# Attention with sinks and two feed-forward layers in one kernel: first tiles' splits, tiny sums, the sinks' values and the last store rearranged

## What is computed

```python
keep = is_sink | in_window            # 4 sinks, window of 128
scores = np.where(keep, scores, -1000000000.0)
a = np.exp(scores - max); a = a / (np.sum(a, axis=-1, keepdims=True) + 1e-09)
x = a @ v                             # batch 2, 8 heads, 768 positions, 64 per head
h = x @ w_in                          # 1536 tokens, 512 -> 1024
sm = e / (np.sum(e, axis=-1, keepdims=True) + 1e-09)      # e = exp(h - h_max)
solu = h * sm
ln = (solu - mu) / np.sqrt(var + 1e-06) * g_ln
x2 = ln @ w_out                       # 1024 -> 512
r = np.maximum(x2 @ w2_in, 0.0)       # 512 -> 2048
out = (r * r) @ w2_out                # 2048 -> 512
```

## Time and profile before

| what | value |
|---|---|
| runs shown | 488.4, 488.94 (median), 490.08 us |
| profiled execution's own time | 489.99 us |
| its span in the trace | 488.0 us |
| PE busy | 474.4 us (97%) |
| DVE busy | 289.5 us (59%) |
| ACT busy | 202.9 us (42%) |
| POOL busy | 95.4 us (20%) |
| DMA moved | 40.75 MB |

### The profile page before, as it was taken

How to read it: one execution, slowest core, us unless ns; L and a number is a source line. 1 busy time by engine, 2 the same in 40 slices (tenths; PEclk the granted TensorE clock), 3 DMA queues, 4 the chain that set the end, 5 groups by cost and what they waited for, 6 DMA issues and landing times.

```text
span 488.0 us, 7178 instructions
## 1 busy us (share of the span) xinstructions
PE 474.4 (97%) x2580; PEld 386.6 (79%) x2580; DVE 289.5 (59%) x528; ACT 202.9 (42%) x531; POOL 95.4 (20%) x138
## 2 busy tenths in 40 slices
PE   7989988999999999999999999999999999999997
PEld 5657767887888888888888888888888888888885
DVE  3999999999999999576655453422223232322232
ACT  3767557655776566323225342422222222222221
POOL 2456043020302330719940000000000000000000
PEclk9999999999999999999999999999999999999999
DMA  8921426675558334196400000200000010000002
GB/s 239 311 54 55 145 59 199 172 211 174 153 162 206 95 103 130 27 263 218 97 1 0 0 1 0 88 0 0 0 0 0 0 63 23 1 0 0 1 1 87
DMA packets 50150, 40.75 MB, mean 84 GB/s; under 512 B 27912, under 2 KB 36104, under 8 KB 49608
## 3 DMA queue, kind: packets, MB, share of 16 engines
q1 hardware_dynamic: 49656, 39.83, 28.0%
q10 hardware_dynamic: 464, 0.53, 0.4%
HBM read 29.86 MB, written 10.49 MB: 83 GB/s over the span
## 4 chain that ended last, share of the span: by engine, by line
PE 85%; DVE 9%; issue 2%; ACT 1%; POOL 1%; DMA 1%; SPq 0%; DVEq 0%; POOLq 0%; ACTq 0%
PE score_ps L1524 27%; PE h_ps L1538 13%; PE w_ps L1365 12%; PE h_ps L1325 10%; PE wt_ps L1538 7%; PE w_ps L1538 7%; PE o_ps L1295 3%; PE score_ps L1267 2%; PE wt_ps L1275 2%; DMA x2T<-kT 1%; PE o_ps L1312 1%; PE wt_ps L1267 1%; DVE nmax L931 1%; DVE prob L996 1%; DVE sm L919 1%
## 5 line engine op out<-in xcount | busy, mean ns | idle before, releaser
L1524 PE MATMUL score_ps<-x2T_hi,w2in_hi 128*128 (+1 forms) x192 | 74.8, 389 | 0.0
L1524 PE MATMUL score_ps<-x2T_hi,w2in_lo 128*128 (+1 forms) x192 | 74.7, 389 | 0.0
L1524 PE MATMUL score_ps<-x2T_lo,w2in_hi 128*128 (+1 forms) x192 | 74.7, 389 | 0.0
L1198 DVE TENSOR_TENSOR e<-e 128x512 f32<-128x512 f32 x24 | 17.1, 712 | 82.1 <-ACT e L865 82.1
L1198 DVE TENSOR_TENSOR sq<-relu 128x512 f32<-128x512 f32 x24 | 17.7, 738 | 77.9 <-ACT relu L865 77.9
L865 ACT ACTIVATE relu<-score_ps 128x512 f32<-128x512 f32 x24 | 14.4, 598 | 94.2 <-PE score_ps L1524 94.2
L865 ACT ACTIVATE e<-score_ps 128x512 f32<-128x512 f32 x24 | 14.4, 599 | 92.5 <-PE score_ps L1524 92.5
L1524 PEld LDWEIGHTS score_ps<-x2T_hi,w2in_lo 128*128 128x128 f32 x192 | 36.1, 188 | 7.5
L1524 PEld LDWEIGHTS score_ps<-x2T_hi,w2in_hi 128*128 128x128 f32 x192 | 36.0, 188 | 7.5
L1524 PEld LDWEIGHTS score_ps<-x2T_lo,w2in_hi 128*128 128x128 f32 x192 | 36.0, 188 | 7.5
L675 ACT ACTIVATE prob<-sm,nbias 128x132 f32<-128x132 f32 (+1 forms) x96 | 37.7, 394 | 0.8
(11 more groups left out here) (185 smaller groups left out, 1096.6 us busy)
## 6 DMA issues: line engine op xcount, KB each, us to landing
w2in<-w_in SPq DMA_DIRECT2D x4, 1024.0 KB, 5.2
u_dram<-uT SPq DMA_DIRECT2D x16, 256.0 KB, 3.3
lnT_raw<-u_dram SPq DMA_DIRECT2D x32, 128.0 KB, 2.6
w2out<-w_out SPq DMA_DIRECT2D x8, 512.0 KB, 8.0
V<-v SPq DMA_DIRECT2D x12, 256.0 KB, 3.3
x2T<-x_dram SPq DMA_DIRECT2D x12, 256.0 KB, 4.6
x_dram<-x SPq DMA_DIRECT2D x44, 64.0 KB, 2.3
k_raw<-kT SPq DMA_DIRECT2D x20, 132.0 KB, 2.8
```

The costliest lines, as they stand in the source:

```text
L1198: nc.vector.tensor_tensor(sq[f % 2], relu[f % 2], relu[f % 2], ALU.mult).then_inc(sq_ready, 1)
L1524: done = mm(h2_ps[f % 2], ws[:, c, fs], xs[:, c, bass.ts(blk, BLK)], start=(c == 0 and i == 0), stop=(c == MC - 1 and i == 2))
```

## The change

What it does, by engine:

- **SP** loads the fourth part of w_in ahead of the sinks' values.
- **ACT** rounds this part before the last copy of tile 1's scores. It takes over the rounding of tile 2's queries and keys from POOL. For every tile it computes hz and hz_eps in two activations on 128x1 (`hidden_sum`), behind the exponentials of h.
- **DVE** splits tile 1's keys only after tile 0's maxima of h, and tile 2's keys between the two gates of tile 0. Its three tiny operations per tile are gone.
- **POOL** computes var in front of rstd (`inverse_std`).
- **PE** takes the sinks' values ahead of the first scores of a step and of the other values, for tiles 3 to 5 and 7 to 11. They now open the accumulation in o_ps, and the rounding of x waits for both kinds. ACT's and POOL's first work of stage B waits for the other values where it waited for the sinks'.
- **The end:** the last block's stores are written out behind the loop; the last tile is copied in halves, of which SP stores one and ACT the other.

```diff
...
+def sinks_lead(n):
...
+    return has_sinks(n) and n > EARLY
...
         minus_half = sbt("minus_half", [P, 1])
+        z_floor = sbt("z_floor", [P, 1])
...
         y_done, y_copied_act, y_copied_dve = sem("y_done"), sem("y_copied_act"), sem("y_copied_dve")
+        y_end_copied = sem("y_end_copied")
...
             load_w_in(2)
+            load_w_in(3)
             load_v_sink(0)
-            load_w_in(3)
...
             load_x2T(2)
-            with sp.Fori(0, NB) as blk:
+            with sp.Fori(0, NB - 1) as blk:
...
                     sp.dma_start(out[bass.ds(blk * BLK + i * P, P), :], y[i]).then_inc(y_stored, 16)
-            sp.wait_ge(y_stored, 16 * TB * NB)
+            for i in range(TB):
+                cols = slice(0, DM // 2 if i == TB - 1 else DM)
+                sp.wait_ge((y_copied_act, y_copied_dve)[i % 2], TB // 2 * (NB - 1) + i // 2 + 1)
+                sp.dma_start(out[(NB - 1) * BLK + i * P:(NB - 1) * BLK + (i + 1) * P, cols], y[i][:, cols]
+                             ).then_inc(y_stored, 16)
+            sp.wait_ge(y_stored, 16 * (TB * NB + 1))
...
             nc.gpsimd.memset(minus_half[:, :], -0.5).then_inc(built, 1)
+            nc.gpsimd.memset(z_floor[:, :], SM_EPS * LN_EPS ** 0.5).then_inc(built, 1)
...
             def inverse_std(t):
+                pool.wait_ge(moments_ready, t + 1)
+                pool.wait_ge(hz_eps_ready, t + 1)
+                nc.gpsimd.tensor_tensor(var[:, :], moments[:, 1:2], hz_eps[:, :], ALU.add).then_inc(var_ready, 1)
...
-            def round_k(n):
-                pool.wait_ge(k_loaded, 32 * (n - 1))
-                pool.wait_ge(k_split, n - 1)
-                nc.gpsimd.tensor_copy(KH[:, :, KEYS_SINKS[n % 2]], raw_keys(n)).then_inc(k_hi, 1)
...
             round_v_sink(0)
-            round_k(2)
-            round_q(2)
...
             halves(1, 1)
+            pool.wait_ge(q_hi, 1)
...
-            pool.wait_ge(o_done, sink_tiles(NT))
+            pool.wait_ge(pv_done, GROUPS * NT)
...
+            def hidden_sum(t):
...
+                act.wait_ge(h_exped, 2 * t + 2)
+                nc.scalar.activation(hz[:, :], hsum[:, 0:1], ACT.Identity, bias=hsum[:, 1:2], scale=1.0
+                                     ).then_inc(hz_ready, 1)
+                act.wait_ge(hz_ready, t + 1)
+                if t:
+                    act.wait_ge(var_ready, t)
+                else:
+                    act.wait_ge(built, 3)
+                nc.scalar.activation(hz_eps[:, :], hz[:, :], ACT.Square, bias=z_floor[:, :], scale=LN_EPS ** 0.5
+                                     ).then_inc(hz_eps_ready, 1)
...
                     act.wait_ge(o_done, sink_tiles(n) + 1)
-                else:
-                    act.wait_ge(pv_done, GROUPS * n + GROUPS)
+                act.wait_ge(pv_done, GROUPS * n + GROUPS)
...
                     hidden_exp(t + 1)
+                    hidden_sum(t + 1)
...
                     hidden_exp(t + 1)
+                    hidden_sum(t + 1)
...
                 copy_sinksT(2)
+                hidden_sum(1)
...
             copy_earlier(1, 2)
+            round_w_in(3)
...
                 softmax_exp(1, h)
-            round_w_in(3)
...
             copy_pT(1, 0)
+            round_q(2)
...
             copy_sinksT(1)
+            round_k(2)
+            hidden_sum(0)
...
             act.wait_ge(lnT_split, len(LN_PARTS) * (NT - 2))
-            act.wait_ge(o_done, sink_tiles(NT))
+            act.wait_ge(pv_done, GROUPS * NT)
...
             hidden_exp(NT - 1)
+            hidden_sum(NT - 1)
...
                 copy_y(blk)
+            act.wait_ge(y_end_copied, 1)
+            act.dma_start(out[T - P:T, DM // 2:DM], y[TB - 1][:, DM // 2:DM]).then_inc(y_stored, 16)
...
                 nc.vector.tensor_tensor(u[:, cols], h_ps[:, cols], e[:, cols], ALU.mult).then_inc(u_ready, 1)
-                if half == 1:
-                    nc.vector.scalar_tensor_tensor(hz[:, :], hsum[:, 0:1], SM_EPS, hsum[:, 1:2], ALU.add,
-                                                   ALU.add).then_inc(hz_ready, 1)
...
-            def variance(t):
-                dve.wait_ge(hz_ready, t + 1)
+            def aggregate(t):
                 dve.wait_ge(bstat_ready, 2 * t + 2)
-                nc.vector.scalar_tensor_tensor(hz_eps[:, :], hz[:, :], LN_EPS, hz[:, :], ALU.mult, ALU.mult
-                                               ).then_inc(hz_eps_ready, 1)
                 nc.vector.bn_aggr(moments[:, :], bstat[:, :, :]).then_inc(moments_ready, 1)
-                dve.wait_ge(hz_eps_ready, t + 1)
-                dve.wait_ge(moments_ready, t + 1)
-                nc.vector.tensor_tensor(var[:, :], moments[:, 1:2], hz_eps[:, :], ALU.add).then_inc(var_ready, 1)
...
                     stats(t, half)
-                variance(t)
+                aggregate(t)
...
                 gate(0, 0)
+                split_k(2)
...
                 stats(0, 1)
-                variance(0)
+                aggregate(0)
...
                 stats(1, 1)
-                variance(1)
+                aggregate(1)
...
             row_max(1, 1)
-            split_k(1)
...
             hidden_max_all(0)
-            split_k(2)
+            split_k(1)
...
                     dve.wait_ge(y_done, TB * blk + i + 1)
-                    nc.vector.tensor_copy(y[i], y_ps[i]).then_inc(y_copied_dve, 1)
+                    if blk == NB - 1 and i == TB - 1:
+                        nc.vector.tensor_copy(y[i][:, 0:DM // 2], y_ps[i][:, 0:DM // 2]).then_inc(y_copied_dve, 1)
+                        nc.vector.tensor_copy(y[i][:, DM // 2:DM], y_ps[i][:, DM // 2:DM]).then_inc(y_end_copied, 1)
+                    else:
+                        nc.vector.tensor_copy(y[i], y_ps[i]).then_inc(y_copied_dve, 1)
...
                         last = mm(o_ps[rows, cols], V[:, slot, h * D:(h + 1) * D], pT[:, g, j * P:(j + 1) * P],
-                                  start=(g == 0 and part == 0 and i < 2),
-                                  stop=(alone(n) and g == GROUPS - 1 and i >= HG - 2), skip_group_check=True)
+                                  start=(g == 0 and part == 0 and i < 2 and not sinks_lead(n)),
+                                  stop=((alone(n) or sinks_lead(n)) and g == GROUPS - 1 and part == len(parts) - 1 and i >= HG - 2), skip_group_check=True)
...
                 pe.wait_ge(p_sinkT_copied, sink_tiles(n) + 1)
+                if sinks_lead(n):
+                    pe.wait_ge(xT_split, n)
...
                     cols = slice(c * P, (c + 1) * P)
-                    last = mm(o_ps[:, cols], v_sink[0:SKS, n // TPB, cols], p_sinkT[0:SKS, :], start=False,
-                              stop=(c == MC - 1), skip_group_check=True)
+                    last = mm(o_ps[:, cols], v_sink[0:SKS, n // TPB, cols], p_sinkT[0:SKS, :],
+                              start=(c == 0 and sinks_lead(n)), stop=(c == MC - 1 and not sinks_lead(n)), skip_group_check=True)
...
                 first = LEAD if t == EARLY else 0
+                if has_sinks(n):
+                    sink_values(n)
...
                 values(n, 1)
-                if has_sinks(n):
-                    sink_values(n)
...
                 n = NT - 1
+                sink_values(n)
...
                 values(n, 1)
-                sink_values(n)
...
```

## The result

The changed kernel took 487.09 us (median of 7 runs, 486.21 to 488.67) where the kernel before took 489.54 in the same comparison (488.4 to 490.23). The ratio is 0.9946, with a 95% interval of 0.993 to 0.9963, which leaves out 1: faster, by 0.54%. The prediction was 486.7 us, between 485.3 and 488.4. The profiled execution took 487.09 us, with a span of 485.4.

What follows compares the result with a forecast made beforehand. PE was taken to bound stage B and the steady steps, DVE the first tiles. Gains of 1.0 + 0.35 + 0.4 + 0.35 + 0.1 = 2.2 us took the median from 488.94 to 486.7 us, range 485.3 to 488.4.

Steps and rivals of the forecast that it cites:

- steady steps: Tiles 4, 5, 7 to 10: fewer stops between forms of product save 0.4 us, bounds 0 and 1.0.
- Part 1: First tiles: the new order of loads, roundings and splits brings tile 1's hidden product 1.0 us earlier, bounds 0.3 and 1.8.
- step 2: Sinks' values fill PE's wait for tile 4's keys, with DVE's tiny sums gone: 0.35 us, bounds 0 and 0.59.
- Rival (a): First tiles give nothing, as DVE's wait for ACT's key rounding or POOL's longer chain takes it; 487.7 us, chance 0.20.
- Part 2, steady steps: Moving tiny sums to ACT and POOL only gives DVE slack in steady steps, since PE is the bound: nothing gained.
- u at 69.98 not 0.5 but 0.35 earlier, held by POOL: In step 2, DVE's merge comes about 0.5 us earlier, but u only 0.35, held by POOL.
- Parts 2 and 3 are both needed there: In step 2, the moved tiny sums and the sinks' values ahead give 0.35 us only together.
- I take 0.06 a step: Steady steps: of PEld's 0.17 us idle ahead of the sinks, part is hidden; 0.06 us saved in each of six steps.
- Rival (c): More gain: PEld's whole 0.17 us goes in six steady steps, first tiles give 1.7; 485.4 us, chance 0.12.
- Rival (b): Slower: DVE's chain, with 0.09 us of slack left, becomes the bound of the steady steps; 490.6 us, chance 0.08.
- Last step: Sinks fill PEld's 0.39 us wait for POOL's mask before tile 11's last values: 0.35 us, bounds 0.15 and 0.5.
- Tail: Last tile in halves, its stores queuing behind earlier ones on busy DMA engines: 0.1 us, bounds -0.2 and 0.4.

Runs made afterwards that it cites:

- e5: Changed kernel with hz, hz_eps and var computed on DVE again; 487.44 us, ratio 0.9948 to the kernel before.
- e7: Changed kernel with tile 2's keys and queries rounded on POOL again, DVE's new order kept; 492.46 us, ratio 1.0063 to the kernel before.
- e2: Kernel before with only hz, hz_eps and var moved from DVE to ACT and POOL; 489.36 us, ratio 0.9993 to the kernel before.
- e3: Kernel before with only the sinks' values taken ahead, the tiny sums left on DVE; 488.15 us, ratio 0.9972 to the kernel before.
- e6: Changed kernel with the sinks' values between a step's first and second scores, two more changes of form; 489.62 us, ratio 0.9988 to the kernel before.
- e9: Changed kernel with x split before u's normalization (steps 2, 5) and tile 4's first two merges before the second statistics (step 2); 486.96 us, ratio 0.9938 to before.
- e12: Changed kernel with x split before u's normalization (steps 2, 5) and step 2's last six output products laid into PE's waits; 485.71 us, ratio 0.991 to before.
- e11: Changed kernel keeping, of its first-tile edits, only w_in's earlier load and rounding; DVE's old order and POOL's roundings back; 488.76 us, ratio 0.9978 to before.

## Why the prediction was right, and where it wasn't

- **Total.** 486.7 was forecast and 487.09 measured; 2.2 us of gain forecast, 2.45 between the medians. The spans differ by 2.6 and, without the chance of the start, by 2.86. That the forecast came within 0.4 us is in part luck: the kernel before took 489.54 us this time, 0.60 more than the 488.94 from which the forecast went out, and this hid part of the gain that was missed. The sum was 0.66 too small: the steady steps alone were 0.66 too low, Part 1 was 0.18 too low and step 2 0.17 too high.
- **Part 1** (1.0 forecast, 1.18 measured) was right by its own steps: second normalization at 25.85 forecast, 26.03 measured, or 25.77 without the later start; the split of w_in 1.35 forecast, 1.21 measured; the new wait 0.2 and 0.15; xT_lo 1.0 earlier and 0.93, or 1.19 without the later start. Two operations that the sum left as they were changed too, and nearly cancel: the split of the sinks' values took 0.68 instead of 1.00, that of tile 2's keys 0.88 instead of 0.70. It was also right to give hz a share of it (0.35 forecast, 0.25 by e5). What it didn't say is that the move to ACT is a condition for the rest as long as POOL rounds ahead of its masks (e7).
- **Rival (a)** had its mechanism, the wait for ACT's rounding, and it exists, but costs 0.15 us.
- **Part 2, steady steps**: nothing forecast, nothing found (e2, e5). POOL's addition took 0.19 in the steps shown, 0.2 assumed; ACT's two took 0.29 each, 0.2 assumed.
- **Step 2** was mis-sized: 0.35 forecast, 0.18 measured. The failed step is "u at 69.98 not 0.5 but 0.35 earlier, held by POOL". Counted from the scores, the aggregation came only 0.16 us earlier (67.74 against 68.85 less the 0.95 that all stands earlier), because hz and hz_eps had overlapped their neighbours: 0.15 us of length each, but under 0.1 of delay. From the aggregation to u it is 1.15 us now and 1.13 before, so u came 0.14 us earlier and not 0.35. The merge, 0.41 earlier, has PE's scores early and nothing else. "Parts 2 and 3 are both needed there" failed too: part 2 alone gives 0.14 (e2), part 3 alone nothing (e3). An operation's length in the timeline isn't the time that its removal gives.
- **Steady steps** are the term that failed most: 0.4 forecast, 1.06 measured, above its upper bound of 1.0. The step "I take 0.06 a step" supposed that much of PEld's 0.17 us is hidden by running products. It isn't: a step with sinks is 0.19 us shorter, and e6 loses 0.42 for two changes of form more. The bound was the idle time of PEld alone and left out the slower first products of the new form. Rival (c) had this term right, 1.0, and the first tiles with 1.7 wrong. (Its sum gives 485.4; the range began at 485.3, which changes nothing.)
- **Rival (b)** said that DVE's chain would have 0.09 us of slack left. It has: xT_lo ends at 134.08 in the steady step above, a waiting product follows such an end by 0.15 us (tile 6's, 117.80 and 117.95), and tile 7's starts at 134.31, so 0.08 us are left. But nothing used them up, not even DVE's own tiny operations (e3, e5); here 0.08 us were enough.
- **Last step** 0.35 forecast, 0.37 measured. The sinks start 0.09 sooner behind the transpositions than the values did, the five groups take 2.38 instead of 2.77 us (0.31 of it is the wait for the mask, and the number of changes of form is two in both), and the first four output products take 0.08 longer behind the values than behind the sinks.
- **Tail** 0.1 forecast, 0.08 here and about 0.1 over all traces. The full DMA engines were the right reason.
- Of the signs named beforehand, two failed. Steady steps repeat in 16.27 and not "in 16.4 us or a little less", on the good side. And "PE waits for xT_lo in no step but step 5" is wrong by step 2, where it waits 0.45 us, which it didn't before: the chain over POOL's rstd and u is what its term there had too fast.

## What to carry to other kernels

On an engine that never waits, count the changes of form between products and put products of one form next to each other; here one change less in a step was worth more than all relief of a neighbour engine. An operation moved late on one engine delays whoever waits to overwrite its input, so look for who frees what before choosing the engine that waits. And an earlier start is only worth what the next late thing allows: look at the wait behind, and lay independent work into it, before making work ahead of it shorter. That both together would pay here is argued: no run has e9's order and e12's filling in one kernel.

## What the runs showed of the hardware

- A change between forms of product (64 rows, 64 columns, full) costs PE about 0.2 us here: 0.19 us between steps with four and five, 0.42 between four and six. From full products to those on 96 rows the trace shows no cost: 0.23 us from one to the next, as between full ones.
- PE's granted clock fell to its lower level (0.50, that is 1.2 GHz; stretches that hold both levels show 0.57 to 0.70) for some 3 us behind waits of 1.32 (e6) and 1.50 us (e9) and behind several waits of up to 1.03 us close together (e11), and for some 7 us from within a wait of 3.80 us on (e7). In the trace of the kernel before it stayed at 1.00 behind a wait of 1.34 us, in every microsecond from 60 to 76. So a wait of the same size cost nothing more in one execution and some 1.3 us at lower speed in another. Over all executions a mean granted clock of 0.997 or less was seen in 8 of 8 of e7, 3 of 5 of e9, 4 of 10 of e11, 5 of 12 of e6, 1 of 12 of e2, 1 of 12 of the changed kernel, none in the other experiments, and 4 of 87 of the kernel before. So these kernels differ in how often it falls; what decides in one execution stays open.
- Where DVE and POOL worked at the same time, one of the two was often longer: DVE's split of w_in took 1.62 to 1.63 us with POOL's rounding beside its start, 1.21 without; its split of tile 1's keys 1.57 beside POOL's addition on 96x512. In the new place POOL was at work beside that split too, and there DVE took 0.70, and POOL's gathering of the sinks' probabilities 0.64 instead of 0.25.
